# Attention weights turned and multiplied in blocks of 128, 128 and 36 lanes that cross the heads

## The reference

```python
k_p = k.reshape(B, H, 72, 8, D).mean(axis=3)         # pooled keys, 72 per head
v_p = v.reshape(B, H, 72, 8, D).mean(axis=3)
scores = q @ k_p.T / sqrt(D);  attn = softmax(scores)   # over 72 keys
x = (attn @ v_p)  as [4608, 512]                     # heads side by side
logits = x @ phi                                     # [4608, 32]
d = softmax(logits, over tokens); slot_input = d.T @ x
slot_out = per expert relu(slot_input @ w1) @ w2
y = softmax(logits, over slots) @ slot_out
h = relu(y @ w_in);  out = (s * h * h + b) @ w_out
```

## Time and profile before

| | before |
|---|---|
| median of 3 runs | 655.31 us |
| profiled execution, its own time | 654.17 us |
| its span | 652.2 us |
| TensorE busy | 628.5 us, 96% |
| TensorE weight loads busy | 544.4 us, 83% |
| VectorE busy | 479.9 us, 74% |
| ScalarE busy | 449.4 us, 69% |
| GpSimd busy | 123.8 us, 19% |
| chain that ended last, share of TensorE | 86% |

### The profile page before, as it was taken

The page is one execution under the profiler, slowest core; times in us unless marked ns, Lnnn a source line. Parts: engine busy times, 40 slices in busy tenths (PEclk is TensorE's granted clock), DMA queues, the critical chain, the costliest instruction groups (busy, mean ns, idle before and its releaser), DMA issues.

```text
span 652.2 us, 16678 instructions
## 1 busy us (share of the span) xinstructions
PE 628.5 (96%) x6462; PEld 544.4 (83%) x6462; DVE 479.9 (74%) x794; ACT 449.4 (69%) x753; POOL 123.8 (19%) x126
## 2 busy tenths in 40 slices
PE   7799999999999999989999999999999999999996
PEld 6577777777753248879999999999999999999996
DVE  5888685566345638976888888888878888888876
ACT  2587767777422169986777777777777777777772
POOL 4787887622110010003100000000000000000001
PEclk9799999999998989999999999999999999999999
DMA  9978979672489960000100000000000000000001
GB/s 333 316 223 329 319 258 401 194 302 119 142 315 428 410 255 1 1 0 26 42 33 19 34 16 32 16 32 16 32 16 16 32 22 26 16 32 16 33 18 65
DMA packets 26004, 80.49 MB, mean 123 GB/s; under 512 B 6496, under 2 KB 14688, under 8 KB 23392
## 3 DMA queue, kind: packets, MB, share of 16 engines
q1 hardware_dynamic: 25952, 79.76, 32.8%
HBM read 70.32 MB, written 9.44 MB: 122 GB/s over the span
## 4 chain that ended last, share of the span: by engine, by line
PE 86%; POOL 3%; DMA 3%; ACT 2%; DVE 2%; issue 2%; SPq 0%; DVEq 0%; ACTq 0%; POOLq 0%
PE bank L1922 16%; PE bank L1912 16%; PE bank L1911 16%; PE bank L1816 5%; PE bank L1674 4%; PE bank L1839 2%; PE bank L1780 2%; PE bank L1842 2%; PE bank L1759 2%; PE bank L1661 2%; PE bank L1846 2%; PE bank L1600 2%; PE bank L1633 2%; DMA kvbuf<-in_v_dram 2%; PE bank L1704 1%
## 5 line engine op out<-in xcount | busy, mean ns | idle before, releaser
L1354 DVE TENSOR_TENSOR lo_sb<-a_sb,hi_sb 128x896 fp32r<-128x896 f32 x128 | 140.1, 1094 | 56.6 <-PE bank L1922 55.5
L1028 ACT ACTIVATE hi_sb<-a_sb 128x896 fp32r<-128x896 f32 x128 | 122.2, 955 | 78.5 <-PE bank L1912 74.7
L1911 PE MATMUL bank<-w_hi,hi_sb 128*128 128x256 f32 x381 | 96.9, 283 | 0.0
L1912 PE MATMUL bank<-w_lo,hi_sb 128*128 128x256 f32 x381 | 96.9, 283 | 0.0
L1013 ACT ACTIVATE a_sb<-r_sb 128x512 f32<-128x512 f32 x144 | 91.1, 632 | 6.5
L1922 PE MATMUL bank<-w_hi,lo_sb 128*128 128x256 f32 x381 | 87.1, 283 | 0.0
L1006 ACT ACTIVATE r_sb<-bank 128x512 f32<-128x512 f32 x144 | 83.6, 581 | 0.0
L1911 PEld LDWEIGHTS bank<-w_hi,hi_sb 128*128 128x128 f32 x381 | 73.2, 192 | 0.0
L1912 PEld LDWEIGHTS bank<-w_lo,hi_sb 128*128 128x128 f32 x381 | 73.2, 192 | 0.0
L843 POOL TENSOR_TENSOR pu_sb<-pu_sb,logits 128x256 f32<-128x256 f32 x1 | 0.7, 738 | 334.5 <-DVE x_sb L1412 334.5
L1912 PE MATMUL bank<-t_early,hi_sb 128*128 128x256 f32 x256 | 64.2, 283 | 0.0
(11 more groups left out here) (210 smaller groups left out, 1304.5 us busy)
## 6 DMA issues: line engine op xcount, KB each, us to landing
early_third<-in_moe_w_dram SPq DMA_DIRECT2D x5, 2048.0 KB, 12.3
kvbuf<-in_k_dram SPq DMA_DIRECT2D x12, 768.0 KB, 5.7
kvbuf<-in_v_dram SPq DMA_DIRECT2D x12, 768.0 KB, 6.6
out_dram<-o_sb SPq DMA_DIRECT2D x36, 256.0 KB, 2.3
qbuf<-in_q_dram SPq DMA_DIRECT2D x8, 1024.0 KB, 9.1
early<-in_moe_w_dram SPq DMA_DIRECT2D x4, 2048.0 KB, 11.1
late<-in_moe_w_dram SPq DMA_DIRECT2D x3, 2048.0 KB, 13.7
after_last<-in_moe_w_dram SPq DMA_DIRECT2D x2, 2048.0 KB, 9.5
```

The costliest lines, as they stand in the source:

```text
L1028: act.activation(hi_sb[:, n % 2, :], a_sb[:, n % ARING, P:2 * CH], ACT.Copy).then_inc(hi_ready, 1)
L1354: dve.tensor_tensor(lo_sb[:, n % 2, :], a_sb[:, n % ARING, P:2 * CH], hi_sb[:, n % 2, :].bitcast(F32), ALU.subtract).then_inc(lo_ready, 1)
L1911: pe.matmul(acc, hi, rhs_hi, start=(k == 0 and (at == AT1 or at % 2 == 1)), stop=False, skip_group_check=True)
L1912: last = pe.matmul(acc, hi, rhs_lo, start=False, stop=False, skip_group_check=True)
```

## The change

- **Blocks.** Four heads' weights with their sum lanes are 4 x 73 = 292 adjacent columns of `ex`. These are now turned in blocks of 128, 128 and 36 columns: six transposes per unit in place of eight. Blocks one and two go to one PSUM bank and are copied at once to `aT` [128, 2, 2, 128], the third to another and to `aT_end` (36 rows).
- **V phi in that form.** `vT` becomes 256 columns wide per pair of heads, zeroed once by VectorE at the start (`vT_zero`, which ScalarE waits for ahead of its first copy): the even head in columns 0 to 71, the odd one in 73 to 144, in their own partitions. So any 128 adjacent columns of it, multiplied by `phi_st` (phi of a pair of heads, one above the other, 32 columns), give V phi in lanes across the heads. The second block straddles two pairs and takes two matmuls that add up. `phi_bd` with its zeroing and its wait goes. ScalarE copies V phi in two parts.
- **Logits.** Per unmixed unit three products (128, 128 and 36 rows) in three quarters in place of four of 72 rows; per mixed unit 12 in place of 16, in the order half, batch, block. `l4` and the fold over it have 96 rows. The mixed unit's heads lie in `ex` in their natural order.
- **Natural V.** The pairs in the wide `vT` are no longer one transpose: each head is a matmul with half of `ident`, eight in place of four.
- Buffers are placed anew.

```diff
@@ V phi, on TensorE
-                for a in range(PH // 2):
-                    last = pe.matmul(bank[Q_B if i else B_B][0:KEYS, 2 * SLOTS * a:2 * SLOTS * (a + 1)], vT[:, a, :], phi_bd[:, a % HP, :],
-                                     start=True, stop=True)
+                for x in range(BLOCKS):
+                    for batch_half in range(4):
+                        at = P * x + SLOTS * batch_half
+                        found = block_values(batch_half, x)
+                        for part, (a, values) in enumerate(found):
+                            last = pe.matmul(bank[Q_B if i else B_B][0:block_rows(x), at:at + SLOTS], values, phi_st[:, a % HP, :],
+                                             start=(part == 0), stop=(part == len(found) - 1))
@@ natural V
                 for a in range(HP):
-                    last = pe.transpose(natural_bank(i, half)[0:KEYS, P * a:P * (a + 1)], vT[:, HP * half + a, :], ident[:, :])
+                    for t in range(2):
+                        at = P * a + HD * t
+                        last = pe.matmul(natural_bank(i, half)[0:KEYS, at:at + HD], vT[:, HP * half + a, lanes_of(t)],
+                                         ident[:, HD * t:HD * (t + 1)], start=True, stop=True)
@@ logits
                     if is_mixed(U):
-                        for g in range(2):
+                        for half in range(2):
                             for bb, toks in parts():
-                                for a in range(HB):
-                                    h = HB * g + a
-                                    last = pe.matmul(bank[L_B][QUAD * a:QUAD * (a + 1), toks], vphi[i % 2][:, H * bb + h, :],
-                                                     aT[:, HB * (h % 2) + h // 2, toks], start=(g == 0 and bb == 0), stop=(g == 1),
+                                for x in range(BLOCKS):
+                                    last = pe.matmul(bank[L_B][QUAD * x:QUAD * (x + 1), toks], vphi[i % 2][0:block_rows(x), x, 2 * bb + half, :],
+                                                     turned_of(x)[:, half, toks], start=(half == 0 and bb == 0), stop=(half == 1),
                                                      skip_group_check=True)
                     else:
-                        for a in range(HB):
-                            last = pe.matmul(bank[L_B][QUAD * a:QUAD * (a + 1), 0:L4], vphi[i % 2][:, H * bb + HB * unit_half(U) + a, :],
-                                             aT[:, :, :].rearrange("k (j a) p -> k a j p", j=2)[:, a],
+                        for x in range(BLOCKS):
+                            last = pe.matmul(bank[L_B][QUAD * x:QUAD * (x + 1), 0:L4],
+                                             vphi[i % 2][0:block_rows(x), x, 2 * bb + unit_half(U), :],
+                                             turned_of(x).rearrange("r j p -> r (j p)"),
                                              start=(unit_half(U) == 0), stop=(unit_half(U) == 1), skip_group_check=True)
@@ turning the weights
-                    for g in range(2):
+                    for g, blocks in enumerate((range(BLOCKS - 1), range(BLOCKS - 1, BLOCKS))):
                         if U:
                             pe.wait_ge(aT_kept, 2 * (U - 1) + g + 1)
-                        for a in range(HB):
-                            last = pe.transpose(bank[A_B[g]][0:KEYS, P * a:P * (a + 1)], ex[:, U % EXR, HB * g + a, 0:KEYS], ident[:, :])
+                        for x in blocks:
+                            for j in range(2):
+                                at = P * (2 * (x - blocks[0]) + j)
+                                lanes = ex[:, U % EXR, HB * j:HB * (j + 1), :].rearrange("p a k -> p (a k)")[:, block_lanes(x)]
+                                last = pe.transpose(bank[A_B[g]][0:block_rows(x), at:at + P], lanes, ident[:, :])
                         last.then_inc(aT_ready, 1)
@@ ScalarE's copies of the turned weights and of V phi
-                    for g in range(2):
-                        act.wait_ge(aT_ready, 2 * U + g + 1)
-                        act.activation(aT[:, HB * g:HB * (g + 1), :],
-                                       bank[A_B[g]][0:KEYS, :].rearrange("p (a g) -> p a g", a=HB), ACT.Copy).then_inc(aT_kept, 1)
+                    rows = block_rows(BLOCKS - 1)
+                    act.wait_ge(aT_ready, 2 * U + 1)
+                    act.activation(aT[:, :, :, :], bank[A_B[0]][:, :].rearrange("r (x j p) -> r x j p", x=BLOCKS - 1, j=2),
+                                   ACT.Copy).then_inc(aT_kept, 1)
+                    act.wait_ge(aT_ready, 2 * U + 2)
+                    act.activation(aT_end[0:rows], bank[A_B[1]][0:rows, 0:2 * P].rearrange("r (j p) -> r j p", j=2),
+                                   ACT.Copy).then_inc(aT_kept, 1)
-                act.activation(vphi[i % 2][:, :, :], bank[Q_B if i else B_B][0:KEYS, :].rearrange("g (h s) -> g h s", s=SLOTS),
-                               ACT.Copy, scale=1.0 / POOL).then_inc(wv_kept, 1)
+                act.activation(vphi[i % 2][:, 0:last], found[:, 0:last], ACT.Copy, scale=1.0 / POOL)
+                act.activation(vphi[i % 2][0:rows, last], found[0:rows, last], ACT.Copy, scale=1.0 / POOL).then_inc(wv_kept, 1)
@@ start: VectorE and GpSimd
+            dve.memset(vT[:, :, :], 0.0).then_inc(vT_zero, 1)
-            pool.memset(phi_bd[:, :, :], 0.0).then_inc(phi_zero, 1)
```

## The result

The median went from 655.75 us (four runs, 654.98 to 659.61) to 681.24 us (four runs, 679.44 to 682.4): the ratio is 1.0374 [1.0327, 1.0421]. The kernel is slower by 25.5 us; 680.3 us stood at the end of the prediction's sum. The profiled execution of after took 682.4 us, its span is 680.6; that of before 654.17 and 652.2.

A forecast was written before the change was run, and what follows sets the result against it. The prediction took TensorE to bound the attention stage. Its terms, -7.9 + 16.6 + 5.0 + 8.4 + 4.6 - 1.7, summed to +25.0 us, a median of 680.3, stated as 680 us; range 670 to 688, by the bounds 675 to 687.

The forecast's parts named there:

- The bound: Attention stage: TensorE sets the pace, so nearly all TensorE time added or taken moves the stage's end.
- the two only tie: Chain of waits at 84 to 92 us: it turns to GpSimd, but TensorE has no wait there.
- Turning: Transposes of attention weights: six for eight save 0.22 us per unit, 36 units, -7.9 us; bounds -7 to -8.
- Logits: Attention logits: the 36-row block runs behind the 128-row ones; +16.6 us for 32 unmixed units, +5.0 for 4 mixed.
- Rival 1: Logits: the third block runs beside the first two, so both logits terms are 0; 659 us, chance 0.12.
- Rival 3: Logits and V phi: each emptying of the array costs more, 96 of them, +10 us; 690 us, chance 0.04.
- Rival 2: Attention stage: TensorE only looks full, the loop through other engines sets a unit's pace; 647 us, chance 0.04.
- V phi: Product of V and phi, once per pair of batches: 3.1 us against 1.03, +8.4 us; bounds 7 to 10.
- Natural V: Transposes of V, twice per pair: eight matmuls for four transposes, 1.03 us against 0.44, +4.6 us; bounds 4 to 5.2.
- ScalarE and the copies: ScalarE's copies of turned weights and V phi: they lie beside TensorE's work nearly everywhere; zero.
- Zeroing: vT's zeroing on VectorE ahead of the first pooling: over by 5.0 us, zero; without cover up to 3.9 us.
- Cover: TensorE's waits before 60 us: of 2.4 us, 1.7 can be filled by added work, -1.7 us.

The follow-up runs named there:

- six turns: The kernel before with six transposes of the attention weights per unit in place of eight, from the third unit on; 652.49 us, ratio 0.9936.
- the turned phi: Kernel before with 128-row blocks for turning and logits, V phi made with phi stationary from the narrow vT, then transposed; 651.68 us, 0.9955.
- the moved matrix: One 2 MB expert matrix load moved behind the last pair's K loads: in the turned phi 655.59 us, in the kernel before 658.98 us.
- whole rows: The changed kernel with the third block's products over all 128 rows, 92 of them zeroed at the start; 661.07 us, ratio 1.0073.
- the mixed unit by block: The changed kernel with the mixed units' loop in the order block, half, batch; 680.42 us, ratio 1.037.
- eight turns: The changed kernel with the third block's two transposes of the attention weights issued twice, so eight per unit; 688.24 us, ratio 1.05.

## Why the prediction was right, and where it wasn't

**The bound.** "Nearly everything that the change adds to or takes from TensorE in this stage moves the end" is half right. It holds for what is added: of +27.7 us of pieces 24.1 arrived in the stage (28.8 with the clock's 4.7), and of 7.6 more 7.0 to 8.3. It does not hold for what is taken away: six turns and the turned phi gave 3.4 of 7.5 and 3.1 of 6.8 us. The earlier trace rows has a hint of it: GpSimd's pieces of the chain from 84 us on, of which the prediction says that "the two only tie". A tie is harmless for a change that adds, and can stop one that saves. That it did so here is argued from the chain of the turned phi (56 to 94 us) and from the moved matrix; the waits without a releaser are the rival, with 2.9 of the 5.3 us more of idle time in six turns and 2.5 of 4.5 in the turned phi. The forecast was right since the change adds.

**Turning.** 0.78 was forecast, 0.80 to 0.81 measured, -7.0 us for -7.9. That is the small end of its bounds; why isn't shown.

**Logits.** The step that carried the forecast, a change of form at 36 rows read off L1704 and L1709 in the earlier trace rows, held to a hundredth: 1.10 and 1.85 us. (8.79 us in 20 rounds is 0.44 us per round, not the 0.43 that the prediction reads off; its sum stays as it is.) "That it is addressed as 64 is my reading" isn't shown as such; shown is that 36 and 128 rows don't run side by side and that 128 and 128 do. Rival 1 needed 0.57 and is out: a unit that would have made it 659 us was built with whole rows, and came to 661. Rival 3 needed some 0.1 us more at each emptying, for which 1.10 and 1.85 have no room. Rival 2 needed TensorE to idle, and it idled for 2.8 of 188.2 us.

**V phi.** 3.00 us for 3.1. Its 24 wide loads at 0.11 us are what sets it: PEld is busy 2.92 of the 3.00 us from 155.60 on, with 32 columns streamed per load. **Natural V**, read off L1532, is 1.03 as forecast (1.03 - 0.44 is 0.59, not the prediction's 0.57; +4.7 us for +4.6).

**ScalarE and the copies.** Timeline of after:

```profile
110.13 0.60 ACT L983 ACTIVATE aT<-bank 128x512 f32<-128x512 f32 x1 [1.15 <-PE bank L1721]
...
110.63 0.36 ACT L986 ACTIVATE aT_end<-bank 36x256 f32<-36x256 f32 x1
...
113.29 0.38 ACT L910 ACTIVATE vphi<-bank 128x256 f32<-128x256 f32 x1 [1.89 <-PE bank L1573]
113.57 0.26 ACT L911 ACTIVATE vphi<-bank 36x128 f32<-36x128 f32 x1
```

The durations are those taken from the earlier trace rows, and V phi's two copies overlap; the engine has idle time ahead of them. TensorE's waits from 24 to 190 us that name ScalarE's copies of V phi are 0.6 us once, against 0.7.

**Zeroing.** VectorE's first 9 us in after:

```profile
1.40 1.76 DVE L1169 MEMSET vT<- 128x2048 f32 x1 [0.35 <-issue]
```

1.76 us, under half of the 3.9 bound, over at 3.2 us and hidden: the first pooling starts at 5.29 us (5.11 before).

**Cover.** Mis-sized: 3.6 us are left over for 1.7. The prediction counted waits up to 60 us only, and said so where it widened the range downwards. It hadn't counted that the stage's idle time behind the first V phi (4.8 us, 2.8 after) would shrink all along.

**The clock.** Not foreseen at all: 4.7 us of the profiled execution. Between the profiled executions the difference is 28.2 us, so the sum of +25.0 was 3.2 us short there: 1.0 from the pieces (27.7 for 26.7) and 4.7 from the clock, less 1.9 of further cover, 0.3 behind the stage and 0.2 outside the span. Between the medians it is 25.5. So it is in part luck that the sum came within 1 us of the median: of the clock's 4.7 us, which the prediction lacked, cover that it counted too low took back 1.9, and after's profiled execution is the slowest of its four. That the range held is no luck, since the terms hold one by one. Half clock stood behind two of four V phi's in after, one of four with whole rows, two of four with the mixed unit by block, and behind the first with eight turns; behind none of before's, six turns' or turned phi's, which take about 1 us. This table by stretches is the mixed-by-block kernel behind its second:

```profile
68.00:71.00 3.00, 3.00 (x30) 1.43 (x22) 2.20 (x4) 1.15 (x2) 0.03 (x1) 0.54 0.88 319
```

So the fall goes with the 3-us V phi of 32 narrow matmuls, though not every time: in these four kernels it stood behind the first V phi each time, but behind only two of the twelve later ones. The first one comes 3 to 7 us after an earlier stretch of half clock that every kernel has (19 to 26 us in after) and has 0.6 us of idle time behind it; before has both of these too (19 to 27 us, 0.7 us), and no fall. What in it brings the fall (streams of 32 columns, a long run of weight loads, the idle time ahead of it) wasn't tried apart and stays open; so is its share in the other executions, since only one of each kernel is profiled.

## What to carry to other kernels

Before you cut matmuls that stand side by side in quarters of the array, ask whether the pieces still have one form: here a 36-row product next to 128-row ones cost more than the product that it saved, and padding it with zero rows to the full 128 brought 20 us back. Narrow results are cheap to stream and dear to load: put the narrow operand on the stationary side and turn the result (1.04 us for 3.00). When you reorder a loop so that forms change less often, look at what it does to the quarters as well: with each quarter's matmuls directly behind one another, two blocks of the mixed unit took 0.82 us where 0.55 was expected. And read a tie in the chain of waits in both directions: added work went through in full here, and less than half of the saved work did.

## What I had not expected of the hardware

- The granted clock fell to half after 3 us of V phi while TensorE was never idle (7.20 of 7.20 us busy at 0.53). It cost 3.0 us there, and 1.7 behind the first V phi, where 0.6 us of idle time stood before it.
- TensorE stalled in the middle of a group of matmuls for 1.55 to 1.85 us with no releaser in the profile, in two kernels that differ from before by a few instructions, and the clock then stood at half for about 3 us (0.50, 0.52). The turned phi has three of 1.0 to 1.3 us. In after the profile shows none of that length. Their cause is open.
- The mixed unit's twelve matmuls took 1.85 us in eight groups of form, 1.38 in two groups with each quarter's matmuls one behind the other (0.82 + 0.56), and 0.58 in one form with the quarters alternating.
